# Attention and two feed-forward layers on one core: the norm's first steps, their mean and a load's wait placed elsewhere

## The reference

```python
cum = np.cumsum(np.log(np.clip(f, 1e-4, 1.0)), axis=-1)
scores = q @ k.T / sqrt(D) + cum[:, None] - cum[None, :]      # causal mask: -1e9
attn = softmax(scores) ; x = attn @ v                          # heads side by side: (2304, 512)
xn = x / sqrt(mean(x * x) + 1e-6) * rms_g
x = (silu(xn @ w_gate) * (xn @ w_val)) @ w_out                 # d_ff 1536
out = silu(x @ w_in) @ w_out2                                  # d_ff 2048
```

## Time and profile before

| | |
|---|---|
| median of three runs | 991.84 us (991.74 to 992.33) |
| profiled execution | 991.74 us, its span 989.7 us |
| TensorE matmul busy | 975.3 us (99%) |
| VectorE, ScalarE, GpSimd busy | 643.1, 449.8, 343.8 us |
| mean granted TensorE clock | 0.998 of full |

### The profile page before, as it was taken

One profiled execution on the slowest core, in us unless ns is written; L12 is line 12 of the kernel. 1 busy time (PEld: TensorE's weight loads), 2 busy tenths in 40 slices (PEclk: granted clock), 3 DMA queues, 4 the chain that ended last, 5 costly groups with the idle time before them and its releaser, 6 DMA issues.

```text
span 989.7 us, 16362 instructions
## 1 busy us (share of the span) xinstructions
PE 975.3 (99%) x5807; PEld 892.2 (90%) x5807; DVE 643.1 (65%) x1259; ACT 449.8 (45%) x961; POOL 343.8 (35%) x326
## 2 busy tenths in 40 slices
PE   8999999899999999999999999999999999999998
PEld 5777777799999999999999999989989899898996
DVE  7787778588758797789682787714837148371441
ACT  6877686445354235344242344523615236152341
POOL 6787766402401553244324243120221202212022
PEclk9999999999999999999999999999999999999999
DMA  7667565277735856668479477242463424624212
GB/s 200 208 193 235 157 188 155 84 262 261 287 128 224 298 196 229 224 244 319 169 275 337 167 290 282 101 168 115 181 252 117 169 111 182 254 110 172 112 34 95
DMA packets 74144, 192.68 MB, mean 195 GB/s; under 512 B 8464, under 2 KB 38928, under 8 KB 67920
## 3 DMA queue, kind: packets, MB, share of 16 engines
q1 hardware_dynamic: 74064, 191.64, 54.0%
HBM read 150.12 MB, written 41.49 MB: 194 GB/s over the span
## 4 chain that ended last, share of the span: by engine, by line
PE 91%; POOL 3%; issue 2%; DVE 1%; ACT 1%; DMA 1%; SPq 0%; DVEq 0%; POOLq 0%
PE banks L1917 20%; PE banks L1918 20%; PE banks L1919 20%; PE banks L2049 7%; PE banks L2050 7%; PE banks L2048 7%; PE banks L1796 4%; PE banks L1748 3%; PE banks L1845 3%; POOL qk_lo L801 1%; ACT probs L987 1%; POOL cum_b L808 1%; DMA cum_b<-cum_dram 1%; PE banks L1819 0%; DMA cum_dram<-zeros 0%
## 5 line engine op out<-in xcount | busy, mean ns | idle before, releaser
L1917 PE MATMUL banks<-xb,wu 128*128 128x384 f32 x864 | 289.5, 335 | 0.0
L1919 PE MATMUL banks<-xb,wu 128*128 128x384 f32 x864 | 289.0, 335 | 0.0
L1918 PE MATMUL banks<-xb,wu 128*128 128x384 f32 x864 | 289.0, 335 | 0.0
L861 POOL TENSOR_TENSOR wd<-stage_d,wd 128x512 fp32r<-128x512 f32 x84 | 119.1, 1423 | 468.2 <-ACT wd L1079 468.2
L1917 PEld LDWEIGHTS banks<-xb,wu 128*128 128x128 f32 x864 | 162.6, 188 | 0.3
L1918 PEld LDWEIGHTS banks<-xb,wu 128*128 128x128 f32 x864 | 162.6, 188 | 0.2
L1919 PEld LDWEIGHTS banks<-xb,wu 128*128 128x128 f32 x864 | 162.5, 188 | 0.0
L1169 ACT ACTIVATE scratch<-scratch 128x384 f32<-128x384 f32 x144 | 75.3, 523 | 113.0 <-DVE scratch L1554 51.2
L1178 ACT ACTIVATE hid_main<-scratch 128x384 fp32r<-128x384 f32 x144 | 72.2, 517 | 118.2 <-DVE scratch L1596 118.2
L1603 DVE TENSOR_TENSOR hid_main<-scratch,hid_main 128x384 fp32r<-128x384 f32 x144 | 88.3, 627 | 40.6 <-ACT hid_main L1178 36.3
L1079 ACT ACTIVATE wd<-stage_d 128x512 fp32r<-128x512 f32 x84 | 51.6, 630 | 135.5 <-PE banks L2050 100.3
(11 more groups left out here) (194 smaller groups left out, 1715.6 us busy)
## 6 DMA issues: line engine op xcount, KB each, us to landing
wu<-kept SPq DMA_DIRECT2D x48, 1792.0 KB, 10.2
stage_d<-w SPq DMA_DIRECT2D x84, 256.0 KB, 2.7
kept<-ws SPq DMA_DIRECT2D x14, 1024.0 KB, 5.2
kept<-wu SPq DMA_DIRECT2D x12, 768.0 KB, 4.1
qk_raw<-qk_t SPq DMA_DIRECT2D x14, 576.0 KB, 3.3
cum_b<-cum_dram SPq DMA_DIRECT2D x30, 256.0 KB, 4.3
kept<-xb SPq DMA_DIRECT2D x6, 1024.0 KB, 5.1
kept<-ws SPq DMA_DIRECT2D x8, 768.0 KB, 6.0
```

The lines of the kernel that those rows point to most:

```text
L861: nc.gpsimd.tensor_tensor(wd[:, d % 2, 1, :], stage_d[:, d % 2, :], f32(wd[:, d % 2, 0, :]), ALU.subtract).then_inc(wd_split, 1)
L1917: nc.tensor.matmul(dst, w_hi_part, m_hi, start=start, stop=False)
L1918: nc.tensor.matmul(dst, w_hi_part, m_lo, start=False, stop=False)
L1919: return nc.tensor.matmul(dst, w_lo_part, m_hi, start=False, stop=stop)
```

## The change

The Newton step of span 0 goes from GpSimd to VectorE, as three instructions for each half in the place of four, put between the two parts of `x_out`. The guess comes one pair later, and ScalarE's order around it is another: `exps` in their usual order, `guess_exp` between the `exps` of tile 3 and the copy of tile 6, `guess_log` ahead of the copy of tile 2. For all pairs `exps(p, 7)` goes behind `row_scales`, and the copy of tile 2 behind what stands at the end of a pair (`w_raw` in pairs 2 and 3, `xb_high` in 15). `first_sums` goes ahead of `row_sums` on GpSimd. TensorE's two halves of the mean go forward, VectorE's copies of them too, and `invert` goes behind the copy of tile 7. SP waits for the landing of `cum_b` for pair 1 before it issues the loads that follow.

```diff
-GUESS_PAIR = 10
-STEP_PAIRS = {11: ((0, 0), (0, 1), (0, 2)), 12: ((0, 3), (1, 0), (1, 1)), 13: ((1, 2), (1, 3))}
+GUESS_PAIR = 11
...
             load_cum(1)
+            sp.wait_ge(cum_in[1], 48)
             load_qk(2)
             load_v(0)
             load_cum_rest(1)
...
@@ gpsimd @@
-            def newton_part(t, k):
...
+                if p in SUMS_PAIRS:
+                    first_sums(SUMS_PAIRS.index(p))
                 if p == PREP_PAIR:
                     w_raw(0)
...
                 row_sums(p)
-                if p in SUMS_PAIRS:
-                    first_sums(SUMS_PAIRS.index(p))
-                for t, k in STEP_PAIRS.get(p, ()):
-                    newton_part(t, k)
...
@@ scalar @@
-                if 0 < p < NPAIRS and p != GUESS_PAIR + 1:
+                if 0 < p < NPAIRS:
                     exps(p, 0)
                     exps(p, 1)
                 if p > 0:
                     take_out(p - 1, 4)
-                if p == GUESS_PAIR + 1:
-                    exps(p, 0)
-                elif 0 < p < NPAIRS:
+                if 0 < p < NPAIRS:
                     exps(p, 2)
                     exps(p, 3)
+                if p == GUESS_PAIR + 1:
+                    guess_exp(0)
...
                     take_out(p - 1, 6)
-                if p == GUESS_PAIR + 1:
-                    exps(p, 1)
-                    exps(p, 2)
-                    exps(p, 3)
...
                     exps(p, 6)
-                    exps(p, 7)
...
-                if p == GUESS_PAIR + 1:
-                    guess_exp(0)
                 if p > 0:
                     row_scales(p - 1)
...
                 if here:
+                    exps(p, 7)
                     exps(p, 8)
-                if 0 < p < NPAIRS:
-                    take_out(p, 2)
                 if p == PREP_PAIR:
                     w_raw(0)
...
                     guess_log(0)
                 if p == NPAIRS - 1:
                     xb_high(0, "B21")
+                if 0 < p < NPAIRS:
+                    take_out(p, 2)
...
@@ vector @@
+                if p in MEAN_PAIRS:
+                    take_first_mean(MEAN_PAIRS.index(p), 0)
                 if here:
                     shift(p, 4)
                     shift(p, 5)
                     shift(p, 6)
                 if p > 0:
-                    invert(p - 1)
                     take_out(p - 1, 7)
                 if p in MEAN_PAIRS:
-                    take_first_mean(MEAN_PAIRS.index(p), 0)
+                    take_first_mean(MEAN_PAIRS.index(p), 1)
+                if p > 0:
+                    invert(p - 1)
                 if here:
                     shift(p, 7)
                 if p > 0:
                     take_out(p - 1, "t1")
-                if p in MEAN_PAIRS:
-                    take_first_mean(MEAN_PAIRS.index(p), 1)
...
                     x_out(p - 1, 0)
-                if p > 0:
-                    x_out(p - 1, 1)
+                if p == GUESS_PAIR + 1:
+                    newton_step(0, 0, 0)
+                    newton_step(0, 0, 1)
+                if p == GUESS_PAIR + 2:
+                    newton_step(0, 1, 0)
+                    newton_step(0, 1, 1)
+                    newton_step(0, 2, 0)
                 if p == GUESS_PAIR + 3:
+                    newton_step(0, 2, 1)
                     normalise_x(0, 0, 0)
                     normalise_x(0, 1, 0)
                 if p == GUESS_PAIR + 4:
                     normalise_x(0, 2, 0)
                     normalise_x(0, 3, 0)
-                if p == GUESS_PAIR + 5:
                     normalise_x(0, 0, 1)
+                if p > 0:
+                    x_out(p - 1, 1)
+                if p == GUESS_PAIR + 4:
                     normalise_x(0, 1, 1)
...
@@ tensor @@
                 both(p - 1, 2)
+                if p in MEAN_PAIRS:
+                    first_mean(MEAN_PAIRS.index(p), 0)
                 scores(p, 2)
                 scores(p, 3)
                 both(p - 1, 3)
                 if p in MEAN_PAIRS:
-                    first_mean(MEAN_PAIRS.index(p), 0)
+                    first_mean(MEAN_PAIRS.index(p), 1)
                 values(p - 1, 0, (0, 1))
                 last_tile(p - 1)
                 scores(p, 4)
-                if p in MEAN_PAIRS:
-                    first_mean(MEAN_PAIRS.index(p), 1)
                 row_factors(p - 1)
```

More of the change, by code:

```diff
@@ L149, in newton_before @@
 def newton_before(span):
-    return 3 * (span - 1)
+    return 0 if span == 0 else 6 + 3 * (span - 1)
 def normed_before(span):
@@ L349, in build @@
         first_turned = sem("first_turned")
-        early_step = sem("early_step")
         out_first = sem("out_first")
@@ L1372, in x_out, with newton_step @@
                                         ALU.mult).then_inc(x_done, 1)
-            def newton_step(span, k):
-                at = newton_before(span) + k
+            def newton_step(span, k, t=None):
+                at = newton_before(span) + (k if t is None else 2 * k + t)
                 if k > 0:
-                    dve.wait_ge(newton, at)
+                    dve.wait_ge(newton, at if t is None else at - 1)
                 else:
@@ L1382, in newton_step @@
                         dve.wait_ge(sums_split, 8)
-                    else:
+                    elif span > 1:
                         dve.wait_ge(hid_split, through(CYCLES_OF[2 * span - 2][-1]))
-                a, b, c = (norm_tmp(span, i) for i in range(3))
+                cols = slice(0, SPAN) if t is None else slice(t * TT, (t + 1) * TT)
+                a, b, c = (norm_tmp(span, i)[:, cols] for i in range(3))
                 if k == 0:
@@ L1396, in normalise_x @@
                 dve.wait_ge(gain_in, 16)
[L1397 to L1400, removed]
+                dve.wait_ge(newton, newton_before(span) + (3 if t is None else 5 + t))
                 cols = slice(0, SPAN) if t is None else slice(t * TT, (t + 1) * TT)
```

## The result

The changed kernel took 1003.49 us in the median (1000.73 to 1003.80), the kernel before 992.0 beside it: a ratio of 1.0109, 95% interval [1.0092, 1.0128]. In a later comparison it was 1003.83 against 991.82, 1.0126 [1.0112, 1.014]. I had forecast 998.9 and 995.0 to 1002.5: the direction was right, the size 4.6 us short, and the range missed it by 1. The profiled execution took 1001.44 (span 999.7), 2 under the median; why such executions differ is part of the answer.

The account below looks back on a forecast made before the run. TensorE was taken to set the pace in attention, each wait paid in full. Terms 0.55 + 0.15 + 3.05 + 1.3 + 1.85 + 0.2 = +7.1 on 991.8 gave 998.9 us, range 995.0 to 1002.5.

Parts of the forecast that it names:

- Pairs 3 and 4: Copy of tile 2 behind w_raw, +0.4; moved reciprocal removes TensorE's 0.23 loss to a late ptb; together +0.15 us.
- The 0.2 for a copy behind w_raw: Pairs 3 and 4: tile 4's transposes wait for ScalarE's later take_out(p, 2), 0.2 us in each, +0.4.
- rival (b): Granted clock falls in the two mean waits; price 1.4 us twice, giving 1001.7; chance 0.12.
- Start: +0.55: SP's wait for cum_b of pair 1: brings up to 0.95, but v comes late, a new wait of 1.5 us.
- Rival (c): At the start, v takes 6.0 us to load and the pair waits 3.5 instead of 1.5: 1000.9; chance 0.12.
- the 0.95: Start: the most SP's wait could win, cum_b's third load landing at 15.0 instead of 15.96 us.
- Mean square: Pairs 9 and 10: TensorE's earlier means wait 2.3 us each, +4.6, less 1.54 of removed waits: +3.05.
- Guess: +1.3: Pair 12: ScalarE's copy behind the Ln and its later copies make TensorE lose 2.0 us, against 0.7 before.
- Newton steps: +1.85: From the end of pair 12: VectorE's steps, blocked by GpSimd's qk split, cost 3.25 us against 1.40.
- rival (a): Ports do not block: Newton steps run in VectorE's idle time, -0.5 instead of +1.85 us, giving 996.5; chance 0.15.
- my 11.0, 11.6 and 11.6: Distances in us between pairs' first transposes forecast for the Newton steps, following one near 12.3 in pair 12.
- End: +0.2: End of attention: normalisings around x_out(14, 1), +0.5 if the fourth is blocked by GpSimd's split, -0.1 if not; taken +0.2 us.

Follow-up runs that it names:

- the fastest version: The kernel before with VectorE's cast ahead of the second take_first_mean, first sums ahead of row_sums, pair 15's last normalisings moved: 985.57 us, -6.25.

## Why the prediction was wrong

1. **Pairs 3 and 4: "the reciprocal behind take_out(p-1, 7) removes the 0.23"; the step failed.** I looked at who waits for ptb and not at who waits for the reciprocal. It releases GpSimd's spread copy and rest_scale, 0.6 later in every pair, into VectorE's cast. Measured: +3.4 alone (0.30 a quiet pair). The 0.2 for a copy behind w_raw was seen once (10.51 instead of 10.31, in the kernels without the late reciprocal) and not twice. The cause is shown: nothing late was made to start earlier when the cast was made to wait, and two thirds of the loss went. That VectorE and GpSimd block one another I had written down for the Newton steps, with its row, and not applied to the other edits. (The Trainium skill, SBUF — State Buffer, "Who interferes with whom", says that copies and casts can enter modes in which VectorE uses the ports that it shares with GpSimd, and can then contend with it. The 1.09 and 1.10 agree with that; whether the cast was in such a mode no row here shows.)
2. **The clock: rival (b), 0.12, with its price of 1.4 twice.** The price was right (1.30 and 1.37), the chance was not: the failed step is that the sum held the two waits at their length only. In the six traces with two such waits unfilled (2.0 to 2.5) the clock fell behind one in two (the changed kernel, the one without SP's wait) and behind both in four, and filling them won 3.7. I had also left out that the new wait for v could do the same (two of eight traces). The length of the wait does not decide by itself: behind waits of 1.48 and 1.49 the clock fell, behind one of 3.03 it did not. For a wait of 2 us the fall must stand in the main sum.
3. **Start: +0.55, measured +2.3.** Rival (c), v in 6.0, was nearer (5.4 and 5.9); I took the median of 16 issues, 4.0, over the one row at this very place. And the 0.95 that the wait could win is there only where cum_dram lands late: in the traces without the wait cum_b was issued from 8.4 to 8.7 us on and the second pair began at 24.9 to 25.3, or it was issued from 9.5 to 9.9 on and the pair began at 25.8 to 26.3 (in one at 27.95: the kernel without SP's wait, with half clock behind a wait of 1.49 for row_min). The one trace I read was of the late sort.
4. **Mean square: waits 2.3 forecast, 2.0 measured; +3.05 forecast.** In the kernel with the waits filled and the reciprocal back the three periods lose 2.3 against the kernel before, 3.0 without the guess that left them: right without the clock. The waits for qk_lo went, as said.
5. **Guess: +1.3.** In that same kernel the pair takes 12.29 us, 2.0 over a quiet one; less the 0.7 of the old guess that is 1.3, as worked out. The medians give 0.6, with intervals that allow either. That the place of the copy behind the Ln was the cause is refuted: with the copy first the wait only moved. I take it that ScalarE's work in one piece is the cause, wherever it stands; no run split it.
6. **Newton steps: +1.85.** Blocked by the qk split, as forecast; rival (a) is out:

```profile
149.83 2.93 POOL L800 TENSOR_TENSOR qk_lo<-qk_raw,qk_hi 128x1280 fp32r<-128x1280 f32 x1 [0.76 <-DVE qk_hi L1272]
...
151.93 1.93 DVE L1363 SCALAR_TENSOR_TENSOR early_tmp<-early_tmp 128x384 f32<-128x384 f32 x2
```

The first step by itself took 1.25, until 153.2, 0.4 behind the end of the split. Periods of 11.01, 11.72 and 11.71 in the kernel without the late reciprocal stand beside my 11.0, 11.6 and 11.6, so 2.1 for the term.
7. **End: +0.2, measured -1.1 to -1.5.** Three normalisings took 3.23 together, where two blocked ones had taken 4.30, and TensorE waited 2.77 instead of 3.18. What it waited for is another copy than I had said. I had looked only at VectorE's take_out(15, 3). The change also puts ScalarE's copy of tile 2 behind `xb_high`, and that waits for a normalising:

```profile
189.32 0.84 ACT L1011 ACTIVATE xb<-x_sb 128x768 fp32r<-128x768 f32 x1 [0.96 <-DVE x_sb L1376]
190.07 0.36 ACT L979 ACTIVATE pta<-banks 128x256 f32<-128x256 f32 x1
...
190.58 1.52 PE L1778 MATMUL banks<-ident,probs 128*128 128x128 f32 x6 [2.77 <-ACT pta L979]
```

VectorE's copy of tile 3 came right behind it, at 190.66: 3.24 after the first transposes, and 4.39 after them in the kernel before. In the kernel without the late reciprocal the end gave back 1.46 of the Newton term's 2.08.

The single effects add to more than the whole: 2.3 + 3.4 + 6.5 (7.05 less 0.6 for its longer waits) + 0.2 + 0.6 = 13.0 against 11.5 and 12.0. Parts overlap, and each has about 1 us of uncertainty; how the 1 to 1.5 split stays open.

## What to carry to other kernels

When an instruction moves, follow what it releases on the other engines and look at what will run beside that in its new place; an engine's free time is no cover if its instruction is held there by another engine's, as rest_scale was (1.09 instead of 0.45). A new wait in a queue delays everything behind it: list it to the end, and take a transfer's duration from the same place. Price a new wait of TensorE of 2 us with the clock, as a term and not as a rival (here 1.3 to 1.4 us, behind ten of twelve mean waits), and fill it with multiplications whose result is overwritten.

## What the runs showed that I had not expected

Either of two colliding instructions can be the one that is held: rest_scale took 1.09 beside a cast of 0.84 that is recorded 0.02 later, but a cast took 1.10 beside a spread copy of 0.61 that began 0.2 earlier. What decides between them no run shows. The same wait of 2.0 was followed by a fall of the granted clock in some executions and not in others. The kernels with such waits scattered by 1.8 to 4.8 us (but the kernel before, without them, by 4.6 in one comparison), while the fastest version, whose longest wait behind the first 15 us is 0.83, scattered by 0.9.
